# One chunk of both batches per stage, in a linear-recurrence attention kernel with two gated MLPs

## What is computed

```python
for t in range(S):                                      # attention: a linear recurrence over time
    cur = einsum('bhd,bhe->bhde', u[None] * kt, vt)
    y[:, :, t] = einsum('bhd,bhde->bhe', rt, state + cur)
    state = wt[..., None] * state + einsum('bhd,bhe->bhde', kt, vt)

x_prev = x shifted by one step                          # first MLP, 384 -> 1024 -> 384
k = maximum((mu_k * x + (1 - mu_k) * x_prev) @ w_k, 0)
r = sigmoid((mu_r * x + (1 - mu_r) * x_prev) @ w_r)
x = r * (k * k @ w_v)

h = gelu(x @ w_in); u, v = halves of h                  # second MLP
v_s = w_sg @ layernorm(v) + b_sg                        # a product over all 768 steps of one batch
x = x + (u * v_s) @ w_out
```

## Time and profile before

| | |
|---|---|
| median of 3 runs | 332.69 us (331.88 to 332.89) |
| the profiled execution | 332.15 us, span 330.4 us, mean granted clock 0.994 |
| TensorE busy | 320.4 us, 97% of the span |
| VectorE, ScalarE, GpSimd busy | 197.7 us (60%), 151.2 us (46%), 97.7 us (30%) |
| chain that ended last | TensorE 88%, VectorE 4%, ScalarE 3%, DMA 2% |

### The profile page before, as it was taken

One profiled execution on the slowest core, in us unless ns is written; L12 is line 12 of the kernel. 1 busy time (PEld: TensorE's weight loads), 2 busy tenths in 40 slices (PEclk: granted clock), 3 DMA queues, 4 the chain that ended last, 5 costly groups with the idle time before them and its releaser, 6 DMA issues.

```text
span 330.4 us, 6795 instructions
## 1 busy us (share of the span) xinstructions
PE 320.4 (97%) x2682; PEld 300.5 (91%) x2682; DVE 197.7 (60%) x331; ACT 151.2 (46%) x301; POOL 97.7 (30%) x94
## 2 busy tenths in 40 slices
PE   6987999999999999999999999999999999999996
PEld 2656989999999999999999998899999989999996
DVE  4879999983696399639417065991643546123432
ACT  6448554544845455465547692755113025311100
POOL 5530343104314201430032050672333018313220
PEclk9999799999999999999999999999999999999999
DMA  7979043142304401300006046000000210000012
GB/s 234 407 260 370 4 137 130 70 138 60 137 3 163 167 4 28 140 9 2 8 10 237 0 131 233 22 0 0 2 0 0 97 49 2 0 0 2 0 48 95
DMA packets 11153, 28.09 MB, mean 85 GB/s; under 512 B 1232, under 2 KB 5872, under 8 KB 9840
## 3 DMA queue, kind: packets, MB, share of 16 engines
q1 hardware_dynamic: 10976, 27.51, 23.6%
q10 hardware_dynamic: 144, 0.14, 0.1%
HBM read 24.74 MB, written 2.36 MB: 82 GB/s over the span
## 4 chain that ended last, share of the span: by engine, by line
PE 88%; DVE 4%; ACT 3%; DMA 2%; issue 1%; POOL 0%; SPq 0%; ACTq 0%; DVEq 0%
PE dense L305 16%; PE dense L306 16%; PE dense L307 15%; PE ps L623 4%; PE pkt L650 3%; PE ps L306 3%; PE ps L307 3%; PE ps L305 3%; PE py L706 3%; PE py L692 2%; PE pu L673 2%; PE pkt L306 2%; PE pkt L305 2%; PE pkt L307 2%; PE pu L306 2%; PE pu L305 2%
## 5 line engine op out<-in xcount | busy, mean ns | idle before, releaser
L550 POOL TENSOR_TENSOR k_l<-sq,k_h 128x512 fp32r<-128x512 f32 x24 | 32.0, 1334 | 79.3 <-ACT sq L962 79.3
L305 PE MATMUL dense<-xkr_h,wk_h 128*128 128x256 f32 x144 | 42.4, 294 | 0.0
L305 PE MATMUL dense<-k_h,wv_h 128*128 128x256 f32 x144 | 41.3, 287 | 0.4 <-POOL k_l L550 0.4
L306 PE MATMUL dense<-xkr_l,wk_h 128*128 128x256 f32 x144 | 40.9, 284 | 0.0
L307 PE MATMUL dense<-xkr_h,wk_l 128*128 128x256 f32 x144 | 40.8, 284 | 0.0
L307 PE MATMUL dense<-k_h,wv_l 128*128 128x256 f32 x144 | 40.8, 283 | 0.0
L306 PE MATMUL dense<-k_l,wv_h 128*128 128x256 f32 x144 | 40.8, 283 | 0.0
L541 POOL TENSOR_TENSOR rkp<-inw 128x512 f32<-128x512 f32 x12 | 15.3, 1282 | 62.2 <-DVE r_in L1149 62.2
L954 ACT ACTIVATE relu<-dense 128x512 f32<-128x512 f32 x24 | 14.3, 596 | 35.8 <-PE dense L307 35.8
L603 POOL TENSOR_TENSOR gated_l<-gf,gated_h 128x384 fp32r<-128x384 f32 x16 | 16.4, 1023 | 46.5 <-ACT gated_h L1072 36.2
L305 PEld LDWEIGHTS dense<-xkr_h,wk_h 128*128 128x128 f32 x144 | 27.8, 193 | 1.0 <-issue 0.3
(11 more groups left out here) (247 smaller groups left out, 884.2 us busy)
## 6 DMA issues: line engine op xcount, KB each, us to landing
inw<-in_units SPq DMA_DIRECT2D x10, 1026.5 KB, 5.0
vb<-in_vT SPq DMA_DIRECT2D x12, 256.0 KB, 5.2
wsg_raw<-in_wsgT SPq DMA_DIRECT2D x1, 2304.0 KB, 8.5
out_y<-y_out SPq DMA_DIRECT2D x12, 192.0 KB, 1.9
wk_raw<-in_moe_w_k SPq DMA_DIRECT2D x3, 512.0 KB, 9.6
wv_raw<-in_moe_w_v SPq DMA_DIRECT2D x4, 384.0 KB, 7.3
win_raw<-in_moe_w_in SPq DMA_DIRECT2D x3, 512.0 KB, 4.7
inw<-in_units SPq DMA_DIRECT2D x2, 512.0 KB, 5.3
```

What stands on the lines that cost most here:

```text
L305: pe.matmul(o, a_h, b_h, start=first and n == 0, stop=False, skip_group_check=True)
L306: pe.matmul(o, a_h, b_l, start=False, stop=False, skip_group_check=True)
L550: pool.tensor_tensor(k2_l[:, 2 * n:2 * n + 2], sq[:, j % 2].rearrange("p (g t) -> p g t", g=2), k2_h[:, 2 * n:2 * n + 2], ALU.subtract).th ...
```

## The change

- Units alternate between the batches: unit `un` is chunk `un // 2` of batch `un % 2`, and a stage is one chunk of both batches. `X` gets a column ahead of each batch's strip; `from_state` is left out for units 0 and 1 (before: 0 and 6), and `carry_on`, `keys_by_step` and `add_state` for 10 and 11 (before: 5 and 11). A unit's state is that of `un - 2`.
- The last columns of units 0 and 1 both go by selection products, none of them by DMA.
- In stage 0 TensorE does K tiles 0 to 2 ahead of the scores of unit 2, and unit 3 behind unit 2, ahead of the V tiles; stage 1 has a list of its own. From stage 2 on TensorE's list is as before.
- Stage 0: two of the four `key_low` go from GpSimd to VectorE; `wk_l[1]` goes into the mixes and `wk_l[2]` behind them. The loads of wv are issued ahead of `choose(0)`.
- The second MLP's split of `x2` for batch 0 has two parts, since the last chunk of batch 0 is ready only in the last stage.

The core of the diff, by engine: common, SyncE, GpSimd, TensorE, ScalarE, VectorE.

```diff
-    STAGES = B * S // T
+    assert B == N
+    STAGES = S // C
...
+        MOVED = range(N)
 
         def bonus_bank(un):
-            return ps[:, 1] if un == 1 else pkt[:]
+            return [py[:], ps[:, 1]][un] if un < N else pkt[:]
...
+            return [ps[:, 0, 0:C], pkt[:, 0:C]][un] if un in MOVED else y_bank(un)[:, MAIN:WIDE]
...
+            return un // N, un % N, un // N
...
-            eng.wait_ge(x_in, 16 * HANDED * (N * (s + 1) - 1))
+            if s:
+                eng.wait_ge(x_in, 16 * HANDED * N * s)
...
+        EARLY = 2
+
+        def key_lows(eng, j):
+
+            eng.wait_ge(k2le_done, min(j, EARLY))
+            if j > EARLY:
+                eng.wait_ge(k2l_done, j - EARLY)
...
+        XSPLIT = [(0, slice(0, S - C), range(STAGES - 1)), (0, slice(S - C, S), range(STAGES - 1, STAGES)),
+                  (1, slice(0, S), range(STAGES))]
...
-            give_output(0)
+            for j in parts_of("wv"):
+                load_part(sp, j)
             choose(0)
             load_unit(3)
             load_v(3)
-            for j in parts_of("wv"):
-                load_part(sp, j)
...
+            pool.wait_ge(sc_mm, 3)
             products(2)
+            pool.wait_ge(rin_done, 4)
             products(3)
-            for n in range(KG - 1):
+            for n in range(EARLY, KG):
                 key_low(0, n)
             products(4)
-            key_low(0, KG - 1)
+            for n in range(2):
+                key_low(1, n)
             products(5)
-            for s in range(1, STAGES):
+            for n in range(2, KG):
+                key_low(1, n)
+            products(6)
+            products(7)
...
+                if flagged is not None:
+                    flag_of(flagged)
...
+            main = range(PAIRS - 1)
+            last = range(PAIRS - 1, PAIRS)
             warm(pe, 4)
             scores(0)
             keys_by_step(0)
+            flag_of(0)
             warm(pe, 1)
             add_state(0)
-            warm(pe, 2)
             scores(1)
-            bonus(0)
-            flag_of(0)
-            from_chunk(0)
-            bonus(1)
-            for pairs, done in ((range(PAIRS - 1, PAIRS), last_mm), (range(PAIRS - 1), y_mm)):
-                from_state(1, pairs)
-                from_chunk(1, pairs, done)
-            move_last(1)
+            for un in range(N):
+                bonus(un)
+                from_chunk(un, last, last_mm)
+                from_chunk(un, main)
+            for un in MOVED:
+                move_last(un)
             keys_by_step(1)
-            pe.wait_ge(y_done, 1)
             pe.wait_ge(main_done, 1)
-            warm(pe, 2)
+            warm(pe, 1)
             for s in range(STAGES):
                 a, b = 2 * s + 2, 2 * s + 3
                 if s == 0:
                     for tile in RS:
                         first_mlp(s, *tile)
                     add_state(1)
-                    first_mlp(s, *KS[0])
+                    for tile in KS[:3]:
+                        first_mlp(s, *tile)
                     scores(a)
                     keys_by_step(a)
-                    first_mlp(s, *KS[1])
+                    first_mlp(s, *KS[3])
                     outputs(a)
                     scores(b)
                     keys_by_step(b)
-                    flag_of(s + 1)
+                    outputs(b, s + 1)
+                    for tile in VS:
+                        first_mlp(s, *tile)
+                elif s == 1:
+                    for tile in RS + KS[:2]:
+                        first_mlp(s, *tile)
+                    scores(a)
+                    keys_by_step(a)
                     first_mlp(s, *KS[2])
-                    outputs(b)
+                    outputs(a)
+                    scores(b)
+                    keys_by_step(b)
                     first_mlp(s, *KS[3])
+                    outputs(b, s + 1)
                     scores(b + 1)
...
+                    if x == 0 or (b == 0 and x == ST - 1):
+                        parts = 3 if b else 2 if x else 1
+                        pe.wait_ge(x2h_done, KT * parts)
+                        pe.wait_ge(x2l_done, KT * parts)
...
             keys(0)
+            flag_out(0)
             high_weight(0)
-            high_weight(wk[0])
-            high_weight(wk[1])
-            flag_out(0)
-            high_weight(wk[2])
+            for j in wk:
+                high_weight(j)
             act.wait_ge(s_par, 16)
             mix(0)
...
+                    high_weight(wv[2])
+                    key_high(s, 1)
+                    high_weight(wv[3])
+                    key_high(s, 2)
+                    keys(a)
+                    key_high(s, 3)
                     check(a)
-                    keys(a)
-                    key_high(s, 1)
-                    high_weight(wv[2])
                     check(b)
                     keys(b)
                     flag_out(s + 1)
+                    mix(s + 1)
...
-                    dve.tensor_tensor(z[:], added, state[:, (un - 1) % 2], ALU.add).then_inc(z_done, 1)
-                    dve.wait_ge(z_done, n - place(un)[1])
+                    dve.tensor_tensor(z[:], added, state[:, un % N], ALU.add).then_inc(z_done, 1)
+                    dve.wait_ge(z_done, n - N + 1)
+                    dve.wait_ge(y_mm, un + 1)
                     added = z[:]
-                dve.tensor_tensor(state[:, un % 2], added, total, ALU.mult).then_inc(state_done, 1)
-
-            def output(un):
-
-                s, _, _ = place(un)
-                values = inw[:, un % 3, VF]
+                dve.tensor_tensor(state[:, un % N], added, total, ALU.mult).then_inc(state_done, 1)
...
-                    if s == 0 and i == KT:
-                        low_part(dve, parts_of("wk")[2], wl2_done)
+                    if s == 0 and i == KT + 1:
+                        low_part(dve, parts_of("wk")[1], wl2_done)
                 mix_low(s, *MIXES[-1])
+                if s == 0:
+                    low_part(dve, parts_of("wk")[2], wl2_done)
+
+            def key_low(n):
+                dve.wait_ge(sq_done, n + 1)
+                dve.wait_ge(k2h_done, n + 1)
+                dve.tensor_tensor(k2_l[:, 2 * n:2 * n + 2], sq[:, n % 2].rearrange("p (g t) -> p g t", g=2),
+                                  k2_h[:, 2 * n:2 * n + 2], ALU.subtract).then_inc(k2le_done, 1)
 
...
+            choose(0)
             dve.wait_ge(s_att, 1)
             mask(0)
-            carry_on(0)
             mask(1)
-            bonus(0)
-            output(0)
-            choose(0)
-            bonus(1)
-            output(1)
+            for un in range(N):
+                bonus(un)
+                last_output(un)
+                if un == 0:
+                    carry_on(0)
+            for un in range(N):
+                main_output(un)
             dve.wait_ge(omu_done, 1)
             mix(0)
-            scan(2)
             carry_on(1)
-            low_part(dve, wv[0], wl2_done)
-            scan(3)
             for s in range(STAGES):
                 a, b = 2 * s + 2, 2 * s + 3
-                if s < STAGES - 1:
-                    if s == 0:
-                        mask(a)
+                if s == 0:
+                    scan(a)
+                    low_part(dve, wv[0], wl2_done)
+                    key_low(0)
+                    mask(a)
+                    key_low(1)
+                    scan(b)
                     bonus(a)
-                    carry_on(a)
                     output(a)
                     mask(b)
-                    if s == 0:
-                        low_part(dve, wv[1], wl2_done)
+                    carry_on(a)
+                    low_part(dve, wv[1], wl2_done)
+                    bonus(b)
+                    low_part(dve, wv[2], wl2_done)
+                    output(b)
+                    choose(s + 1)
+                    low_part(dve, wv[3], wl2_done)
+                    mix(s + 1)
+                    carry_on(b)
+                    for tile in VS:
+                        value(s, *tile)
+                    scan(a + 2)
+                elif s == 1:
+                    scan(b)
+                    mask(a)
+                    bonus(a)
+                    output(a)
+                    carry_on(a)
+                    mask(b)
+                    scan(a + 2)
+                    bonus(b)
+                    output(b)
+                    carry_on(b)
+                    mask(a + 2)
+                    choose(s + 1)
+                    mix(s + 1)
+                    scan(b + 2)
+                    for tile in VS:
+                        value(s, *tile)
```

More of the change, by code:

```diff
@@ L1088, in plain_recurrence, with plain_batch @@
                 dve.sem_clear(p_init)
-                with dve.Fori(0, (c0 + N) * C // STEPS):
+                for b in range(B):
+                    if b:
+                        dve.memset(p_state[:], 0.0).then_inc(p_zero, 1)
+                        dve.wait_ge(p_zero, 1)
```

(27 more changed lines are left out.)

204 lines of the change are left out of this document (107 added, 97 removed).

## The result

| | before | changed |
|---|---|---|
| median of 8 runs each, same chip | 332.66 us | 331.23 us (330.91 to 331.56) |
| ratio, 95% interval | | 0.996 [0.9947, 0.9972] |
| profiled execution | 332.15 us | 331.37 us |
| its span | 330.4 us | 329.5 us |

The change is faster by 1.4 us, 0.4%. The direction is as forecast and the time lies just inside the range (331.4), but the gain is a third of the 4.1 us forecast.

The account below looks back on a forecast made before the run. Time was taken as the first dense product's moment plus TensorE's work, waits and lost clock. Terms -2.3 - 2.1 - 1.7 - 0.4 + 0.95 + 1.45 = -4.1 gave a median of 328.6 us, range 326.4 to 331.4.

Parts of the forecast that it names:

- First dense product, -2.3: Start of stage 0: selection products replace unit 0's two DMAs, so TensorE's first dense product comes at 22.05, not 24.37.
- Stall, -2.1: Stage 0: TensorE's 2.1 us wait before scores of unit 2, on VectorE's scan, goes.
- Clock, -1.7: Stage 0, behind that wait: the 3.41 us at clock 0.50 go, which gains half of them, 1.7 us.
- Both losses go: Stage 0 at scores(2): the wait and the lowered clock both vanish, counted as -2.1 and -1.7 us.
- Rival one: Before the first dense product: TensorE's 1.5 us idle still lowers the clock, price 1.7 us, time 330.2; chance 0.14.
- Switches and from_state: Stages 0 and 1: fewer starts of dense products behind small ones, -0.4; one extra from_state for unit 6, +0.95 us.
- New waits, +1.45: Stage 0: TensorE newly waits for k_tok at bonus(3) 0.7, the flag behind it 0.6, and wk_l[2] 0.15 us.
- an unbroken TensorE: Stage 1: sign that the forecast is right, TensorE running there without waits.
- Both hold, by 0.4 and 1.4 us: Stage 1: R tile 1's value(V0) is ready 0.4 us early, the scan for scores(4) 1.4 us early; no waits.
- the one meeting shown cost 0.6 to 0.9: Argument against rival two: the one VectorE meeting with GpSimd in the profile cost 0.6 to 0.9 us, not 1.3.
- Rival two: Stage 0: VectorE is the bound, delaying scores(3) or stage 1's R tile 1; 331.2 to 332.7 us; chance 0.10.
- the near end of two: The faster end of rival two's 331.2 to 332.7 us, which the range up to 331.4 was drawn to include.

Follow-up runs that it names:

- the first experiment: The kernel before with two warm products of constants added in TensorE's wait in front of scores(2), nothing else: 331.99 us, ratio 1.0001 to the kernel before.
- the version with all four edits: The changed kernel with two stage-1 key_lows on VectorE, value(V0) ahead of carry_on(3), two GpSimd waits, and from_state(3) ahead of bonus(3): 328.93 us, ratio 0.9908.
- the next kernel: The changed kernel with unit 0's last columns by DMA again and the loads of wv issued behind that hand-over: 333.61 us, ratio 1.0047 to the kernel before.

## Why the prediction was right and wrong

**First dense product, -2.3: right**, 2.0. The mixes started at 20.19, not 19.9. SyncE's loads of wv cost nothing there, but for a reason that I had not named: with a DMA left in that stretch TensorE waits 7.9 us for its first dense product, against 3.7 with these loads behind it.

**Stall, -2.1: right.** The wait is gone, which gave 2.25; scores(2) start at 33.83 unheld (forecast 33.05).

**Clock, -1.7: wrong in kind.** "Both losses go" added two losses that lie under one cover. In the kernel before the next thing that TensorE needs is mask(2), on VectorE, at the same moment whatever the clock; the first experiment gives it back, and from scores(2) to from_chunk(2) 0.05 us are gained. In most executions of the kernel before the clock hadn't fallen at all. I read one execution's clock as the kernel's, and didn't ask what stands behind the slow stretch. The profiles do show a gain of 1.57 from scores(2) to bonus(2), near the 1.7. Against this one execution of the kernel before the number came out, by luck: it is kept only because the change's mask is done when from_chunk(2) wants it, and that is VectorE's queue, not the clock. So the cause was wrong, but this term isn't what put the sum off.

**Rival one, the clock falls all the same: did not come.** TensorE was idle for 1.59 us, and all 8 executions show 1.000. The other kernels, by the idle time of their profiled execution: 2.1 us in the kernel before, and the clock fell in 14 of 57 executions; 3.0 us, in 8 of 8; 3.7 us, in 10 of 12; 7.9 us, in 5 of 5.

**Switches and from_state: right**, -0.5 and +0.97.

**New waits, +1.45: this is the step that failed**; it measured 4.2. The 2.8 between are nearly all of what separates -4.1 from the -0.9 of the spans. In stage 0 it was 2.3 against 1.45: the two that I named came at 0.92 and 0.44, forecast 0.7 and 0.6, with the state product blocked as forecast (1.15); wk_l[2] was 0.47, not 0.15; and each wait costs 0.1 to 0.25 more than its idle time, which I nowhere counted. In stage 1, where I forecast "an unbroken TensorE", it was 2.0 against 0. "Both hold, by 0.4 and 1.4 us" used 2.7 for the hand-over, which took 3.6, with outputs(3) a further 0.9 late (why the hand-over took longer, no run tests); and the scan of unit 5, which stands ahead of mask(4), and r_in of unit 6 have no price there at all, though I had just used the lock for stage 0. GpSimd's rkp waits for r_in, and the change puts two k_l right behind it: the same collision, three times. And "the one meeting shown cost 0.6 to 0.9" had overlooked one: in the kernel before r_in of unit 4 took 1.76 beside a k_l, 1.07 more than alone. Without GpSimd's k_l there k_in and r_in are back at 0.69, and the version with all four edits, without any wait in stage 1, is 1.7 us faster than the change by ratio and 2.5 by profile.

On the lock itself the Trainium skill ("SBUF — State Buffer", on the shared port pair) says that the later of the two is blocked fully for the other's instruction, and the trace agrees: k_in 1.60 and r_in 1.76 against 0.69 each, and both back at 0.69 once GpSimd's operations were elsewhere.

**Rival two**, VectorE the bound, with a chance of 0.10, is the nearest to what happened: its price, 331.2 to 332.7, holds the result, and R tile 1 is where it named it. Its place in stage 0 is wrong: both new key_lows on VectorE took 0.68, near the 0.6 of the forecast, and scores(3) weren't held. That the time still lies in the range of the forecast is no merit of the sum, for the range was drawn to take in "the near end of two".

## What to carry to other kernels

A wait and a slow clock next to each other are one loss if the same engine's next result covers both: before you count the second, find what TensorE needs right behind it, and look whether the clock falls in every execution. When an order is changed, list for every moved stretch what GpSimd does beside VectorE's operations with two inputs in SBUF, in each stage and not only in the one you work on, and look through the whole old timeline for such meetings. Where an edit that removes a wait gains nothing, try it with the edit of the next wait on the same queue before you drop it.

## What was not expected of the hardware

- A lowered clock is not a property of the kernel: of 57 executions of one program 14 had it, and they weren't the longer ones.
- VectorE's scan with two inputs collides with GpSimd as well, 1.91 against 1.23, and both sides pay: two k_l 3.90 against 2.49.
- Two 24 KB transfers behind 1.5 MB of loads on one queue took 9.2 us from issue to use (16.85 to 26.10), against 5.0 in the next kernel, without those loads ahead (issued at 17.26, used at 22.26).
- Each short wait of TensorE costs 0.1 to 0.25 us beyond the idle time that the profile lists. Part of it is in the rows: dense products that follow one another start each 0.12 us though each is listed with 0.28, and that overlap is missing at a wait.
